# Score matmuls of a chunked linear attention: one 128x128 matmul per chunk on masked copies, or four 64x64 array tiles that read the queries in place

## The reference

```python
batch, n_heads, seq, head_dim = (2, 8, 768, 48)
state = zeros((B, H, D, D))
for t in range(S):
    kt, vt, rt, wt = (k[:, :, t], v[:, :, t], r[:, :, t], w[:, :, t])
    cur = einsum('bhd,bhe->bhde', u[None] * kt, vt)
    y[:, :, t] = einsum('bhd,bhde->bhe', rt, state + cur)
    state = wt[:, :, :, None] * state + einsum('bhd,bhe->bhde', kt, vt)
# then: x = y as (batch, seq, 384)
# u = x + real(fft(fft(x, axis=1), axis=2)); u = u + relu(norm(u) @ w_ch1) @ w_ch2
# out = u + gated MLP(u) with GELU, a norm, a 768x768 spatial product, and w_out
```

## Time and profile before

| | |
|---|---|
| median of 2 runs | 490.26 us (490.24 to 490.28) |
| profiled execution, whole | 492.54 us |
| its span in the trace | 490.2 us |
| first score matmul (L964) | at 10.97 us |
| first matmul of the Fourier block (L942) | at 158.96 us |
| one attention iteration | 35.87 us |
| L964 on PE in all | 672 records, 82.9 us busy |
| L500 on ACT in all | 49.7 us from RW, 8.6 us from STG |

### The profile page before, as it was taken

One profiled execution on the slowest core, in us unless ns is written; L12 is line 12 of the kernel. 1 busy time (PEld: TensorE's weight loads), 2 busy tenths in 40 slices (PEclk: granted clock), 3 DMA queues, 4 the chain that ended last, 5 costly groups with the idle time before them and its releaser, 6 DMA issues.

```text
span 490.2 us, 8582 instructions
## 1 busy us (share of the span) xinstructions
PE 453.5 (93%) x2936; PEld 441.0 (90%) x2936; DVE 299.1 (61%) x490; ACT 182.5 (37%) x350; POOL 204.3 (42%) x212
## 2 busy tenths in 40 slices
PE   1798889889887999799999999999999999999997
PEld 1798789789787999799999999999989999989997
DVE  4897997996985587817322232231159866389572
ACT  3766766766760323111121221111145621167120
POOL 2996895995995747817910000000010701006000
PEclk9999999999999599989999999999999999999999
DMA  8942702703400643694400000000000000200002
GB/s 300 384 203 98 265 0 96 265 0 100 197 0 0 234 176 133 219 379 146 161 0 0 0 0 0 0 1 1 1 0 2 0 1 17 80 3 0 1 0 96
DMA packets 8678, 43.64 MB, mean 89 GB/s; under 512 B 1104, under 2 KB 3024, under 8 KB 6864
## 3 DMA queue, kind: packets, MB, share of 16 engines
q1 hardware_dynamic: 7648, 30.36, 16.9%
q0 software_dynamic: 1008, 12.99, 6.9%
HBM read 40.99 MB, written 2.36 MB: 88 GB/s over the span
## 4 chain that ended last, share of the span: by engine, by line
PE 57%; DVE 1%; issue 0%; ACT 0%; ACTq 0%; DVEq 0%
PE PS L942 19%; PE PS L944 18%; PE PS L943 18%; PE PS L1064 1%; PE PS L1052 1%; DVE ME L772 1%; DVE BN L766 0%; DVE HL L812 0%; DVE OUT L929 0%; DVE X L764 0%; ACT HH L589 0%; DVE BN L777 0%; DVE MV L768 0%; ACTq L597 0%; DVEq L771 0%
## 5 line engine op out<-in xcount | busy, mean ns | idle before, releaser
L964 PE MATMUL PS<-RM,KW 128*128 128x128 f32 x672 | 82.9, 282 | 22.3 <-ACT RM L500 13.4
L964 PEld LDWEIGHTS PS<-RM,KW 128*128 128x128 f32 x672 | 78.8, 194 | 25.9 <-issue 21.7
L812 DVE SCALAR_TENSOR_TENSOR HL<-PS,HH 128x384 fp32r<-128x384 f32 x48 | 26.5, 556 | 95.0 <-ACT HH L589 94.9
L589 ACT ACTIVATE HH<-PS 128x384 fp32r<-128x384 f32 x48 | 23.4, 492 | 121.0 <-PE PS L944 113.4
L463 POOL COPY XB<-X 128x384 f32<-128x384 f32 x12 | 6.2, 534 | 147.5 <-PE PS L1064 147.5
L500 ACT COPY RM<-RW 64x384 f32<-64x384 f32 x96 | 49.7, 517 | 17.4 <-POOL RW L386 14.7
L942 PE MATMUL PS<-W2H,HH 128*128 128x384 f32 x144 | 49.1, 341 | 2.3 <-DVE HL L812 2.3
L386 POOL TENSOR_TENSOR RW<-RW,WP 128x384 f32<-128x384 f32 x48 | 49.8, 1054 | 1.9 <-ACT RM L500 1.9
L942 PE MATMUL PS<-UTH,W1H 128*128 128x384 f32 x144 | 48.7, 338 | 0.6 <-DVE UTL L795 0.6
L944 PE MATMUL PS<-W2H,HL 128*128 128x384 f32 x144 | 48.7, 339 | 0.0
L943 PE MATMUL PS<-W2L,HH 128*128 128x384 f32 x144 | 48.7, 338 | 0.0
(11 more groups left out here) (135 smaller groups left out, 1069.6 us busy)
## 6 DMA issues: line engine op xcount, KB each, us to landing
STG<-rkw_dram SPq DMA_DIRECT2D x8, 1152.0 KB, 7.4
RKT<-rk_dram SPq DMA_DIRECT2D x4, 1152.0 KB, 5.3
RAW<-w_dram SPq DMA_DIRECT2D x6, 768.0 KB, 4.4
VST<-v_dram SPq DMA_DIRECT2D x4, 864.0 KB, 4.5
W1H<-w_dram POOLq DMA_DIRECT2D x1, 2304.0 KB, 9.8
W2H<-w_dram POOLq DMA_DIRECT2D x1, 2304.0 KB, 14.6
SGH<-w_sgt_dram POOLq DMA_DIRECT2D x1, 2304.0 KB, 11.7
RAW<-w_sgt_dram SPq DMA_DIRECT2D x3, 768.0 KB, 4.2
```

The costliest lines, as they stand in the source:

```text
L589: act.activation(HH[:, f % HSLOT, :], PS[:, 2 + f % 3, 0:TC], ACT.Relu).then_inc(s_hh, 1)
L812: dve.scalar_tensor_tensor(HL[:, f % HSLOT, :], PS[:, 2 + f % 3, 0:TC], 0.0, HH[:, f % HSLOT, :].bitcast(F32), ALU.max, ALU.subtract).then ...
L964: last = pe.matmul(scores(lev, j)[:, c * C:(c + 1) * C], KW[:, j, c * C:(c + 1) * C], RM[:, j, lev % 2, c, :, :], start=True, stop=True)
```

## The change

RM, `right_blocks` and s_rm are dropped. The score of a chunk is made in four pieces, head `a` by half chunk `b`: weights are 64 partitions by 64 keys of KW, the moving operand is the 32 right-block columns of RW (or STG) in place, and the result goes to PSUM partitions 64b to 64b+63, in the bank of head `a`. At level 6 only the product of the first half's keys with the second half's queries is made, two matmuls a chunk with 64 columns. PSUM is set to zero once at the start, since parts of the score region are no longer written. POOL's product in place (L386) now waits for s_scores, where it waited for s_rm; PE waits for s_upr, where it waited for s_rm. AT has head before chunk. PE's loop over `i` is written out four times.

```diff
@@ PSUM @@
         def scores(lev, j):
             at = 4 * (lev % 2) + 2 * j
-            return PS[:, at:at + 2, :].rearrange("p x n -> p (x n)")[:, 0:NC * C]
+            return PS[:, at:at + 2, 0:NC * C // 2].rearrange("p a (c n) -> p a c n", c=NC)
@@ SP @@
-                sp.wait_ge(s_rm, i * (4 * NLEV) + 4 + START)
+                sp.wait_ge(s_scores, i * (2 * NLEV) + 2 + START)
@@ POOL, ahead of the product of RW @@
                             pool.wait_ge(s_upr, step - 1 + START)
-                            pool.wait_ge(s_rm, i * (4 * NLEV) + 4 * lev + 2 * j + 2 + START)
+                            pool.wait_ge(s_scores, step + 1 + START)
@@ ACT @@
-            def right_blocks(i, lev, j):
-                length = 1 << lev
-                for a in range(2):
-                    rows = slice(HOLD * a, HOLD * (a + 1))
-                    src = STG[rows, j, 0, :] if lev == 0 else RW[rows, j, :]
-                    act.copy(RM[rows, j, lev % 2, :, a, :].rearrange("p c (m l) -> p c m l", l=length),
-                             src.rearrange("p (c m two l) -> p c m two l", c=NC, two=2, l=length)[:, :, :, 1, :]
-                             ).then_inc(s_rm, 1)
...
-                for lev in range(1, NLEV):
-                    for j in range(2):
-                        step = i * (2 * NLEV) + (2 * lev + j)
-                        act.wait_ge(s_upr, step - 1 + START)
-                        if lev >= 2:
-                            act.wait_ge(s_scores, step - 3 + START)
-                        right_blocks(i, lev, j)
-                        if lev == MASKED + 1:
-                            move(MASKED, j)
+                for j in range(2):
+                    move(MASKED, j)
@@ DVE, at the start @@
-            dve.memset(RM[:, :, :, :, :, :], 0.0).then_inc(s_rm0, 1)
+            for at in range(0, 8, 4):
+                dve.memset(PS[:, at:at + 4, :], 0.0).then_inc(s_ps0, 1)
@@ PE @@
+            def score_tile(lev, j, c, a, b):
+                half, length = C // 2, 1 << lev
+                rows, at = slice(HOLD * a, HOLD * (a + 1)), c * C + b * half
+                right = (STG[rows, j, 0, at:at + half] if lev == 0 else RW[rows, j, at:at + half]
+                         ).rearrange("p (m two l) -> p m two l", two=2, l=length)[:, :, 1, :]
+                return pe.matmul(scores(lev, j)[b * half:(b + 1) * half, a, c, b * half // 2:(b + 1) * half // 2],
+                                 KW[rows, j, at:at + half], right, start=True, stop=True)
-            with pe.Fori(0, NIT) as i:
+            pe.wait_ge(s_ps0, 2 + START)
+            for i in range(NIT):
...
-                        pe.wait_ge(s_rm, i * (4 * NLEV) + 4 * lev + 2 * j + 2 + START)
+                        if lev == 0:
+                            pe.wait_ge(s_rkw[j], i * 16 + 16 + START)
+                        else:
+                            pe.wait_ge(s_upr, step - 1 + START)
...
                         for c in range(NC):
-                            last = pe.matmul(scores(lev, j)[:, c * C:(c + 1) * C], KW[:, j, c * C:(c + 1) * C],
-                                             RM[:, j, lev % 2, c, :, :], start=True, stop=True)
+                            if lev < NLEV - 1:
+                                for b in range(2):
+                                    for a in range(2):
+                                        last = score_tile(lev, j, c, a, b)
+                            else:
+                                for a in range(2):
+                                    rows = slice(HOLD * a, HOLD * (a + 1))
+                                    last = pe.matmul(scores(lev, j)[0:half, a, c, :], KW[rows, j, c * C:c * C + half],
+                                                     RW[rows, j, c * C + half:(c + 1) * C], start=True, stop=True)
                         last.then_inc(s_scores, 1)
```

More of the change, by code:

```diff
@@ L154, in build @@
         cursor[0] = masks_at
-        AT = sb("AT", [P, 2, NC, 2, C])
-        RM = sb("RM", [P, 2, 2, NC, 2, C // 2])
+        AT = sb("AT", [P, 2, 2, NC, C])
         MASK = sb("MASK", [P, MASKED, C // 2])
@@ L198, in build @@
         s_v = sem("s_v")
-        s_at0, s_rm0 = sem("s_at0"), sem("s_rm0")
-        s_rm = sem("s_rm")
+        s_at0, s_ps0 = sem("s_at0"), sem("s_ps0")
         s_copied = sem("s_copied")
@@ L493, in _ @@
         def _(act):
-            def right_blocks(i, lev, j):
-                length = 1 << lev
-                for a in range(2):
-                    rows = slice(HOLD * a, HOLD * (a + 1))
-                    src = STG[rows, j, 0, :] if lev == 0 else RW[rows, j, :]
-                    act.copy(RM[rows, j, lev % 2, :, a, :].rearrange("p c (m l) -> p c m l", l=length),
-                             src.rearrange("p (c m two l) -> p c m two l", c=NC, two=2, l=length)[:, :, :, 1, :]
-                             ).then_inc(s_rm, 1)
-            act.wait_ge(s_rm0, 1 + START)
             with act.Fori(0, NIT) as i:
@@ L509, in _ @@
                     act.copy(KW[:, j, :], STG[:, j, 1, :]).then_inc(s_copied, 1)
-                    right_blocks(i, 0, j)
                 for j in range(2):
@@ L524, in move @@
                         rows = slice(2 * m * length, (2 * m + 1) * length)
-                        act.copy(AT[rows, j, :, :, (2 * m + 1) * length:(2 * m + 2) * length].rearrange("p c a l -> p (c a) l"),
-                                 scores(lev, j)[rows, :].rearrange("p (q m l) -> p q m l", q=2 * NC, l=length)[:, :, m, :]
-                                 ).then_inc(s_moved, 1)
-                for lev in range(1, NLEV):
-                    for j in range(2):
-                        step = i * (2 * NLEV) + (2 * lev + j)
-                        act.wait_ge(s_upr, step - 1 + START)
-                        if lev >= 2:
-                            act.wait_ge(s_scores, step - 3 + START)
-                        right_blocks(i, lev, j)
-                        if lev == MASKED + 1:
-                            move(MASKED, j)
+                        act.copy(AT[rows, j, :, :, (2 * m + 1) * length:(2 * m + 2) * length],
+                                 scores(lev, j)[rows, :, :, m * length:(m + 1) * length]).then_inc(s_moved, 1)
+                for j in range(2):
+                    move(MASKED, j)
                 move(NLEV - 1, 0)
@@ L681, in _ @@
                             dve.tensor_tensor(
-                                AT[:, j, :, :, :].rearrange("p c a (m two) -> p (c a) m two", two=2)[:, :, :, 1],
-                                scores(lev, j).rearrange("p (q m) -> p q m", q=2 * NC),
-                                MASK[:, 0:1, :].broadcast_to([P, 2 * NC, C // 2]), ALU.mult).then_inc(s_picked, 1)
+                                AT[:, j, :, :, :].rearrange("p a c (m two) -> p (a c) m two", two=2)[:, :, :, 1],
+                                scores(lev, j), MASK[:, 0:1, :].broadcast_to([P, 2 * NC, C // 2]), ALU.mult).then_inc(s_picked, 1)
                         elif lev < MASKED:
                             dve.copy_predicated(
-                                AT[:, j, :, :, :].rearrange("p c a (m two l) -> p (c a) m two l", two=2, l=length)[:, :, :, 1, :],
+                                AT[:, j, :, :, :].rearrange("p a c (m two l) -> p (a c) m two l", two=2, l=length)[:, :, :, 1, :],
                                 MASK[:, lev:lev + 1, :].bitcast(I32).rearrange("p x (m l) -> p x m l", l=length
                                                                               ).broadcast_to([P, 2 * NC, C // 2 // length, length]),
-                                scores(lev, j).rearrange("p (q m l) -> p q m l", q=2 * NC, l=length),
+                                scores(lev, j),
                             ).then_inc(s_picked, 1)
@@ L996, in _ @@
                         for a in range(2):
-                            last = pe.matmul(y, AT[:, j, c, a, :], VST[:, j, c, a:a + 2, :], start=a == 0,
+                            last = pe.matmul(y, AT[:, j, a, c, :], VST[:, j, c, a:a + 2, :], start=a == 0,
                                              stop=c == 0 and a == 1)
```

## The result

The changed kernel takes **511.49 us** (median of 2 runs, 509.05 and 513.92), the kernel before 490.26: a ratio of 1.0433 with an interval of 1.0219 to 1.0647. Four more runs beside new runs of the kernel before gave 512.2 us and 1.0401 [1.0366, 1.0437]. So it is slower by about 20 us, where 72 were forecast; the range, 497 to 610 us, held it.

What follows compares the result with a forecast made beforehand. Bound: the chain through PE, DVE and POOL, not PE alone. Slower steps and late POOL make iterations 52.4 us for 35.87: +65 over four, less 1 at start included; clock +7; 490.2 + 72 = 562 us, range 497 to 610.

Steps and rivals of the forecast that it cites:

- T: PE's time for one score step of 48 small pairs, levels 0 to 5: forecast 2.74 us, before 1.37.
- B: Rival: four tiles work side by side, T at most 1.5, the late POOL remains; 498 to 504 us; 22%.
- The late POOL: POOL's products wait for PE's scores; end of level 5 to first output takes 12.7 us for 9.1, +3.6 an iteration.
- The clock: Half clock behind PE's gap of about 4 us ahead of the first output: 1.7 us an iteration, +7 us.
- rival C: Small pairs have a floor, or tiles leave PE at half clock through the scores; T 3.2 to 5.5, 580 to 690 us; 18%.
- their gain is nothing: PE's written-out loop drops counters, which lie beside running matmuls: no gain.
- Covered: Zeroing PSUM on DVE at the start hides in its wait for PE; PE's earlier start gives -1 us once.
- The sum: Iteration of 52.4 us for 35.87; four, less 1 at the start, +65, with the clock +72: 562 us.
- A: Forecast case: weight loads of the score tiles follow each other, T from 2.2 to 3.2, 530 to 597 us; 45%.
- D: T at or under 0.7, POOL's lateness free since DVE's L675 runs faster without ACT's copies; 476 us; 6%.

Runs made afterwards that it cites:

- x1: Changed kernel, but ACT copies the right blocks again, unmasked, once a step; tiles read the copy and POOL waits for it: 498.21 us, 1.0114.
- x4: Changed kernel plus 14 idle matmuls an iteration on PE, ahead of the first wait for a state at the outputs: 505.69 us, 1.0295.
- x15: x1 with PE's list as a hardware loop, as in x14: 493.27 us, 1.0023 against the kernel before.
- x16: x15 with the loads of the Fourier tables issued behind POOL's first iteration: 488.79 us, 0.9959 against the kernel before.
- x3: Changed kernel with score matmuls reordered so that six on one array tile follow each other: 587.49 us, 1.1988.
- x2: Kernel before, full-width matmuls and masked copies, with only POOL's wait changed to PE's scores instead of ACT's copy: 526.48 us, 1.0724.
- x14: Changed kernel with PE's list as a hardware loop, waits against counters standing on a semaphore step of PE: 509.27 us, 1.036.
- x7: Kernel before with only PE's loop over the iterations written out: 491.89 us, 1.0001.
- x17: Kernel before with the loads of the Fourier tables issued behind POOL's first iteration: 492.43 us, 1.0012.
- x8: Changed kernel with two array tiles for four, chunks split by head only, 64 partitions by 128 keys: 536.91 us, 1.0918.
- x12: x9 plus two full-width matmuls of 128 columns at the head of each step from level 2 on: 543.29 us, 1.1072.
- x9: Changed kernel with x1's copy, PE's hardware loop and one matmul of a single column heading each step: 516.12 us, 1.0501.

## Why the prediction was right or wrong, point by point

The direction was right, and the time was wrong by 51 us. PE's timelines show where the attention's time went. Per run, the four iterations summed, in us: the scores of levels 0 to 5, from the first matmul of level 6 to the first output with states, and from there to the next scores (after the last iteration to the Fourier block).

| | first score | levels 0 to 5 | level 6 to first output | outputs | first Fourier matmul |
|---|---|---|---|---|---|
| before | 10.97 | 82.5 | 35.8 | 29.7 | 158.96 |
| changed | 9.80 | 82.7 | 47.5 | 38.0 | 178.00 |
| x1, copy | 10.19 | 83.8 | 41.6 | 29.8 | 165.43 |
| x4, gap filled | 9.80 | 86.5 | 47.1 | 30.5 | 173.89 |
| x15, copy and loop | 10.53 | 82.1 | 37.7 | 30.6 | 161.01 |
| x16, and late tables | 10.53 | 79.0 | 36.1 | 31.1 | 156.76 |

By the prediction's steps:

**T, wrong, and all of the miss.** "I see no pair closer than 0.11 us to another", so "loads that are half as long but follow each other": 2.74 us. It is 0.65 at the full clock and 1.25 to 1.5 at the half one. With T = 2.74 the levels 0 to 5 were to take 32.9 us an iteration for 20.0, four times +12.9, or +52 us of the 72. Measured is +0.2. x3 shows that the rule behind it was right for one tile (0.042 us a pair) and wrong for four by turns (0.014). Every row of the kernel before was of one tile, so none could bear on this; and 0.057 was too long even for one tile. The Trainium skill's page TensorEngine Tiling (Array Packing), section Tiling Modes, which the prediction set against itself under B, has tiles load and multiply in parallel, and x3 beside the changed kernel agrees. The Trainium skill's page TensorEngine Tiling (Array Packing), section Performance Considerations, has about 60 cycles for a short matmul, an estimated 0.025 us at 2.4 GHz. By records the trace is under that, 0.014 us from one to the next; by matmuls of the code, two records each, it is 0.028. Counted in that way the Trainium skill's figure would have given a step of 0.6 us by estimate, close to the 0.65 measured; the prediction counted records.

**The late POOL, right in kind, a little too large.** The tail from the end of level 5 to the first output is 88.84 - 77.07 = 11.8 us against 12.7, the gap 3.37 against about 4; most of the difference is L391, 2.76 us for 3.39. Forecast were 3.6 us an iteration, 14.4 in all; the table has 47.5 - 35.8 = 11.7. x1 takes 5.9 of these back. The rest is not the late POOL: two of x1's iterations have 9.3 and 9.2 us there, as before, and the two with 10.9 and 12.2 have matmuls at the half clock there, the second of them also waits for instructions of up to 1.15 us. x2 shows that on full-width matmuls the wait also costs in the levels, 3.0 us an iteration; in the changed kernel the levels as a whole lose nothing.

**The clock, right where it was forecast, and not forecast where most of it was.** Forecast was a fall behind each gap ahead of the outputs, 3.5 us long, 7 us of time in all. The outputs took 38.0 - 29.7 = 8.3 us longer; with x1, where the gap is gone, and with x4, where it is filled, they take 29.8 and 30.5. But of the 76 us at half clock (14 before) only some 17 lie there. Nearly all others lie in the scores, with PE busy, as rival C had it, though not with C's T. What they cost no run has priced. T at half clock is that of the step before, and the levels 0 to 5 take no longer than before, so it may be little.

**"their gain is nothing", of the counters that the written out loop drops: wrong sign.** Writing the loop out costs 5 us in the kernel with the copy (x15) and perhaps 3 in the changed one (x14). With 48 pairs a step the list of instructions is long, and in the first iteration PE stood waiting for it every 126 to 127 pairs; x7 shows that six matmuls a step don't suffer.

**Bulk loads over the instructions, not thought of.** x16 against x15 is 3 to 4.5 us (ratios 1.0023 and 0.9959, medians 493.27 and 488.79), and x17 shows that it isn't the loads' place as such.

**Covered, right.** The zeroing of PSUM, two of 1.76 us, is done at 5.16 us, ahead of anything. PE began at 9.80 us for 10.97, the forecast -1. ACT's copies are gone, and its busy time fell from 182.5 to 124.4 us.

**The sum.** Without T's 52 the forecast has 14.4 for the late POOL, 7 for the clock and -1 at the start, 20 us. Measured in the attention are 11.7, 8.3, -1.2 and 0.2 in the levels, 19.0 us. That the levels come out even is partly chance: shorter steps on PE are paid back by waiting for instructions, 10.9 us, and by the half clock. With the copy, the loop and the late tables (x16) the levels take 3.5 us less than before. Undoing the parts one behind the other took off 14 us (copy), 5 (loop) and 3 to 4.5 (tables). That these add up to the whole is no proof of their sizes, since each is a difference to the run before it, and a part of the clock is in each.

**Rivals.** B was the one that held, T at most 1.5, at 22%: its prices were 498 to 504. It left the clock out; with the prediction's own 7 us its upper price is 511, which is what was measured, though by parts that happen to balance. A at 45% rested on rows that could not speak on it. D expected DVE's product to be shorter without ACT's copies. It is, 0.734 us for 0.914, but x2, which keeps the copies, has 0.703, and x1, with a copy and POOL let go early, 0.891: it seems to go with POOL's waiting, not with the copies.

## What to carry to other kernels

Dropping a copy also drops the buffer that let the writer of its source run ahead: count what the copy released, at every turn of the loop, and then what the new gap does to the clock behind it. Small matmuls on different array tiles overlap when neighbours in the list use different tiles. Several times as many instructions then have to come from memory; here a hardware loop and large loads kept out of the first iteration gave some 5 and 3 to 4.5 us. A row of the profile says nothing on a form of work that it doesn't hold; the width of the chances has to say so.

## What the runs showed of the hardware

- Four 64x64 tiles by turns, 32 columns in f32: 0.014 us from pair to pair at 2.4 GHz, 0.026 to 0.03 at 1.2; one tile only, 0.042 and 0.072. Two 64x128 tiles with 64 columns: 0.056 and 0.107 (x8).
- The granted clock fell to 0.50 with PE busy 5.89 of 6.00 us in such tiles, and stayed at 1.00 with full-width matmuls at 8.22 of 10 us (x2). Dense matmuls of full width set in between (x12) didn't lift it. Why it fell is open.
- From small tiles to one full-width matmul of a single column and back took 0.51 us at the half clock (x9). Two pairs with full-width weights are 0.42 us there by themselves, so the turn costs little, by this estimate.
- Behind a gap of 2.7 to 3.4 us of PE ahead of the outputs the granted clock was 0.66 to 0.80 in them, and they took 8.5 to 10.2 us; with a gap of 0.2 to 0.5 (x1) or a filled one (x4) it was 1.00, and they took 6.8 to 7.1.
- In the first iteration the tiles had the half clock's spacing (x16: 240 pairs in 7.17 us, 0.03 each) with 1.00 in the clock's column. So had x15's 20 full-width records at 41.79 us, 3.79 us for the 2.43 of x16, and the first 24 of the kernel before, 4.36 us for the 2.93 of the next 24. So it is not of the tiles alone, and the column may leave out falls this early; that stays open. The times at half clock given above don't hold it.
- PE waited up to 2.8 us at a time for its instructions, once in 126 to 127 pairs, in the first iteration. The DMA engines were full in two of the three waits of the changed kernel (a share of 1.00 from 17.50 us and 1.03 from 23.80 us), but at 0.28 in the third, from 29.80 us. Later waits were shorter, 0.2 to 1.3 us, the longest with no DMA traffic. So full DMA engines go with long waits, and are not all of the cause.

```profile
23.80:25.80 2.00, 0.01 (x1) 0.00 (x0) 1.92 (x3) 0.00 (x0) 0.64 (x1) 1.00 1.03 422
```
